# Hash-masked attention and two dense layers: transposes, value products and folds each trail the scores by one tile more

## The reference, cut to what matters

```python
q_bits = (np.einsum('bhsd,dk->bhsk', q, proj) > 0)   # k alike
mask = q_bucket[:, :, :, None] == k_bucket[:, :, None, :]
scores = np.where(mask, scale * np.matmul(q, k.transpose(0, 1, 3, 2)), -1e9)
attn = np.exp(scores - max); attn = attn / (sum + 1e-9)
x = np.matmul(attn, v)                  # to (1536, 512)
x = g1(x @ w_in1) @ w_out1              # g1: clipped square
out = (h - np.tanh(h)) @ w_out2         # h = x @ w_in2
```

## Time and profile before

| | |
|---|---|
| median of 3 runs | 764.22 us (764.16 to 764.26) |
| the profiled execution, its own time | 764.02 us |
| its span in the profile | 762.2 us |
| TensorE matmul busy (PE) | 749.6 us, 98% |
| TensorE weight load busy (PEld) | 635.6 us, 83% |
| VectorE (DVE) | 427.3 us, 56% |
| ScalarE (ACT) | 342.9 us, 45% |
| GpSimd (POOL) | 290.0 us, 38% |

### The profile page before, as it was taken

How to read it: one execution, slowest core, us unless ns; L and a number is a source line. 1 busy time by engine, 2 the same in 40 slices (tenths; PEclk the granted TensorE clock), 3 DMA queues, 4 the chain that set the end, 5 groups by cost and what they waited for, 6 DMA issues and landing times.

```text
span 762.2 us, 11644 instructions
## 1 busy us (share of the span) xinstructions
PE 749.6 (98%) x3712; PEld 635.6 (83%) x3712; DVE 427.3 (56%) x743; ACT 342.9 (45%) x679; POOL 290.0 (38%) x226
## 2 busy tenths in 40 slices
PE   5999999999999999999999999999999999999998
PEld 3889989989988888888888888888888888888886
DVE  5999999999995664343433677762221322232223
ACT  5888888888884333343333333342121312222222
POOL 6677977977989991000000465650000000000000
PEclk9999999999999999999999999999999999999999
DMA  7545445544324231000000123210000100010001
GB/s 273 149 134 144 126 130 139 134 128 133 109 77 149 70 124 56 1 0 1 1 0 1 52 86 111 83 56 1 1 0 1 55 0 0 0 55 1 1 0 56
DMA packets 21320, 50.27 MB, mean 66 GB/s; under 512 B 4814, under 2 KB 6990, under 8 KB 21290
## 3 DMA queue, kind: packets, MB, share of 16 engines
q1 hardware_dynamic: 21146, 49.47, 21.2%
q10 hardware_dynamic: 144, 0.39, 0.1%
HBM read 42.04 MB, written 3.19 MB: 59 GB/s over the span
## 4 chain that ended last, share of the span: by engine, by line
PE 85%; DVE 9%; ACT 3%; issue 2%; DMA 1%; DVEq 0%; ACTq 0%
PE ps L667 29%; PE ps L586 29%; PE ps L577 8%; PE ps L563 8%; DVE g_raw L901 5%; PE ps L549 4%; PE ps L552 4%; PE ps L505 2%; DVE g_mid L898 1%; ACT g_hi L777 1%; ACT g_mid L771 1%; DVE clamped L826 1%; DVE p_lo L843 1%; DMA qk_raw<-qk 1%; ACT probs L713 0%
## 5 line engine op out<-in xcount | busy, mean ns | idle before, releaser
L586 PE MATMUL ps<-x_hi,w 128*128 128x512 f32 (+1 forms) x768 | 251.9, 389 | 0.0
L909 DVE TENSOR_TENSOR g_lo<-g_raw,g_hi 128x512 fp32r<-128x512 f32 x96 | 70.9, 738 | 243.3 <-ACT g_hi L777 243.3
L777 ACT ACTIVATE g_hi<-g_raw 128x512 fp32r<-128x512 f32 x96 | 60.7, 632 | 289.9 <-PE ps L667 226.1
L586 PEld LDWEIGHTS ps<-x_hi,w 128*128 128x128 f32 x768 | 144.2, 188 | 29.6
L586 PE MATMUL ps<-x_lo,w 128*128 128x512 f32 (+1 forms) x384 | 149.4, 389 | 0.0
L667 PE MATMUL ps<-g_hi,w 128*128 128x512 f32 x384 | 125.8, 389 | 0.2 <-DVE g_lo L909 0.2
L667 PE MATMUL ps<-w,g_hi 128*128 128x512 f32 x384 | 118.1, 389 | 0.0
L843 DVE TENSOR_TENSOR p_lo<-ps,p_hi 128x384 fp32r<-128x384 f32 x192 | 97.9, 552 | 11.9 <-ACT p_hi L723 11.5
L367 POOL TENSOR_SCALAR w<-stage 128x1024 fp32r<-128x1024 f32 x32 | 37.3, 1166 | 164.3 <-PE ps L667 163.8
L723 ACT ACTIVATE p_hi<-ps 128x384 fp32r<-128x384 f32 x192 | 84.3, 489 | 31.2 <-PE ps L563 30.1
L826 DVE TENSOR_SCALAR_CACHE_REDUCE clamped<-ps 128x768 f32<-128x768 f32 x96 | 91.1, 950 | 1.3 <-ACT probs L713 0.6
(11 more groups left out here) (59 smaller groups left out, 854.7 us busy)
## 6 DMA issues: line engine op xcount, KB each, us to landing
stage<-weights SPq DMA_DIRECT2D x32, 512.0 KB, 3.3
q_raw<-qq SPq DMA_DIRECT2D x16, 384.0 KB, 4.0
k_raw<-kk SPq DMA_DIRECT2D x16, 384.0 KB, 4.9
qk_raw<-qk SPq DMA_DIRECT2D x15, 384.0 KB, 3.9
v_raw<-v SPq DMA_DIRECT2D x16, 192.0 KB, 4.0
inv_wide<-factors SPq DMA_DIRECT2D x16, 192.0 KB, 4.3
out<-stage SPq DMA_DIRECT2D x12, 256.0 KB, 2.1
q_a<-q_b SPq DMA_DIRECT2D x14, 192.0 KB
```

What stands on the lines that cost most here:

```text
L586: last = nc.tensor.matmul(ps[:, f % H_BANKS, :], w[:, f, wp, k * P:(k + 1) * P], xs[:, k, bass.ds(t * TOK, TOK)], start=(k == 0 and wp == ...
L777: nc.scalar.activation(g_hi[:, slot, :], g_raw[:, slot, :], ACT.Copy).then_inc(g_hi_ready, 1)
L909: nc.vector.tensor_tensor(g_lo[:, slot, :], g_raw[:, slot, :], g_hi[:, slot, :].bitcast(F32), ALU.subtract).then_inc(g_split, 1)
```

## The change

Three constants are each one larger:

```diff
-TRANSPOSE_LAG = 4
-PV_LAG = 8
-FOLD_LAG = 10
+TRANSPOSE_LAG = 5
+PV_LAG = 9
+FOLD_LAG = 11
 FACTOR_LAG = 8
 SCALE_TURNS = [8, 10]
```

## The result

The change makes the kernel slower, by more than was forecast. The median of five runs is 772.56 us (770.21 to 773.87) against 764.23 (764.16 to 765.34, five runs); the ratio is 1.0106, with a 95% interval of 1.0095 to 1.0118. The forecast was 769.7 with a range of 765.8 to 771.6, so the sign was right and the size was not. The profiled execution took 773.49 us, 9.47 more than the one of before.

The account below looks back on a forecast made before the run. Nearly full TensorE (27.98 of 27.98 us a pair) and VectorE (26.48) were taken as the bound. Terms 4.0 + 1.5 + 0 = 5.5 us on 764.02 gave 769.5, plus 0.20 for the median: 769.7 us, range 765.8 to 771.6.

Parts of the forecast that it names:

- the mechanism of the loop: Loop: scores start at the later of 2.06 us after the last scores or 1.37 after `parts_lo` two turns before.
- The fold into turn 8: Pairs 1 to 6: fold lands ahead of inversion and clamp of turn 9; 0.67 us a pair, 4.0 us.
- The fold into turn 2: Pairs 1 to 6: later fold delays inversion and the clamp of turn 3; 0.25 us a pair, 1.5 us.
- The fold into turn 11: Loop: fold moves from turn 10 with no inversion near; cost nothing, up to 0.55 us without cover.
- The prediction's own sign of being wrong: Loop: wrong if a pair stays at 28.0 us or grows in turns other than those named.
- The ramp: Pair 0 and drain: taken as nothing; at best 1.27 us returns, at worst twice a clamp's 0.95 is lost.
- The clock: Rival: pauses in the loop drop TensorE to the 1.2 GHz level, 21 us in six pairs, 785 to 790; chance 0.02.
- GpSimd: Loop: its queue comes 1.7 us later, absorbed by its 4.9 us wait, which shrinks to about 3.2; cost nothing.
- Pair 7: Last pair, without bit products: gains and losses net to about nothing, between -0.7 and +0.7 us.
- one unkind ramp: Range's upper end: the sum with 1.9 us added for a bad ramp, 771.6.
- the lesser cost: Rival: only one of the two fold places costs in full; 1.6 to 4 us, 766 to 768; chance 0.20.

Follow-up runs that it names:

- a_factor7: Changed kernel with the inversions one turn earlier, in turns 7 and 1 (FACTOR_LAG 7 instead of 8): 767.25 us, ratio 1.0024.
- b_tr5: Kernel before with the transposes alone one tile later (TRANSPOSE_LAG 5): 783.91 us, ratio 1.0250.
- a_copiesfirst: Changed kernel with SyncE's early loads reordered: bit products' rows, then second head's copies, pair 1's first head last: 770.37 us, ratio 1.0079.
- after_again: The changed kernel as it is, run again in later rounds against the kernel before: 772.37 us, ratio 1.0111.

## Why the prediction was right or wrong

**The direction and the mechanism of the loop: right.** Scores start 1.37 after `parts_lo` of two turns before, or a turn's 2.06 after the last scores. This held in the changed kernel, in the one before and in a_factor7 (pairs 1, 2 and 4), outside the turns that bit products stretch and TensorE's turns next to the jump back. In b_tr5 the waits of the value products come on top.

**The fold into turn 8: right in place and nearly in size.** Forecast 0.67 in each of six pairs; measured 0.71, so 4.3 for 4.0 us (turn 10 of six pairs, 12.61 and 16.86). The fold's own row is 0.55 us, but the next instruction stands 0.58 behind it, and the inversion took 0.50.

**The fold into turn 2: right.** Forecast and measured 0.25 a pair, 1.5 us.

**The fold into turn 11: wrong, and this is the step that failed in the loop.** The prediction said "Cost nothing", since no inversion is near and the distance to turn 2 is the same. But turn 1 grew by 0.25 on average: 13.94 us in six pairs, where it was 12.40, so 1.5 us. It took an inversion to be needed for a loss. In turn 11 the fold stands right ahead of VectorE's jump back, whose 0.19 us are added to it; the forecast did not look at the jump. Where no jump follows, behind pair 6, the move cost nothing, as forecast. A fold alone is no safe place either: in turn 8 it cost 0.25 (a_factor7). In the loop of the kernel before, TensorE's own pause of 0.2 us at its jump back came just behind the fold of turn 10 and covered it. Turns 11 and 0 got shorter by 0.46 us in all. The prediction's own sign of being wrong came true here: a pair grew in a turn that it had not named.

**The ramp: wrong, by the largest amount.** The prediction took "nothing" for it, with at worst a queue behind a later clamp. It looked at engines alone. The step that failed is that the bit products of turn 5, which do not trail, come earlier when the work ahead of them moves back. The prediction didn't ask whether their rows were there. Pair 0 and the drain are 2.85 us longer in the profiled execution: 1.92 of waiting, and the slower clock on top. The engines alone gave what was forecast: with both landings served, pair 0 is 1.62 us shorter than before and the drain 1.4 longer. By the medians of the change and a_copiesfirst the landings cost 2.0 us. Of the change's 8.3 us at the median, 6.1 are left with the landings served, nearly all in the loop.

**The clock: a rival with 0.02, which did take part.** It was priced in the loop, where pauses of 0.7 us left it at 1.00, as forecast. In pair 0 it fell behind 1.92 us without work (the change) and 2.35 us (a_factor7); it stayed at 1.00 behind 1.28 us (after_again) and 1.05 us (b_tr5). The Trainium skill ("TensorE: Matmul & The Clock Gate", Part 1) says that an idle array falls to half its clock; the trace now agrees, with a granted clock of 0.50. Three of the nine runs of the change had a mean granted clock of 0.998 or less, and they are the three longest (773.49, 773.62 and 773.87 us). No edit separates the clock's part from the wait's, so its share of the 2.0 us is not shown.

**GpSimd: right.** Its delay ended in its own wait. That shrank to 3.9 us and not to the forecast 3.2. Counted from the scores of turn 9, `scale_x` starts 2.1 us later than before, but the scores that end the wait come 1.15 us later too. **Pair 7: right**, +0.09. Its parts came as forecast: turn 5 gave back 0.72 us (3.19 to 2.47), turn 4 took 0.25, and turn 10 took 0.55, where 0.48 was forecast. Nothing in the dense layers moved: the last row's 1.37 us is what pair 0 was to give up.

**The range** ended at 771.6. It held one unkind ramp of 1.9 us and no more folds that cost. Its lower end, 765.8, is called the middle of the lesser cost, but 764.2 + 1.6 is that rival's lower end; the middle is 767.0. With the measured terms the sum is 764.2 + 4.3 + 1.5 + 1.1 + 2.0 = 773.1, within a us of the median; 1.1 is the loss in turn 1 less the gain in turns 11 and 0.

One thing stays open: turn 1 of pair 2, the first after the loop's first jump back, takes 2.5 to 2.6 us in every kernel with folds in turn 11, and 2.3 in the pairs behind it. In the change VectorE's wait ahead of that clamp is 0.48 us there, and 0.18 to 0.20 at the later jumps. Why the first one is longer is not shown.

## What to carry to other kernels

A step that trails can't be moved alone: list, for each engine's queue, which of the unmoved steps it now stands in front of, and count it as free only in a turn whose length something else already stretches. Look at the loop's jump back as a step of its own in each queue. The steps that don't trail come earlier in the ramp, so ask of each of them whether its data has landed by then. Where two engines are nearly full, an instruction of half a us may cost half of itself in each round, though its engine shows slack over the whole loop.

## What the runs showed of the hardware that I had not expected

- TensorE idle for 1.92 us in pair 0 was followed by the 1.2 GHz level: 0.66 and 0.50 granted in two stretches of 2 us. In a_factor7 it was idle for 2.35 us, and the clock 0.90, 0.50 and 0.74. After 1.28 and 1.05 us idle at the same place, the clock stayed at 1.00.
- With the DMA engines full, the same load in the same order landed anywhere from 17.41 to 19.45 us in six executions. Ahead of the 768 KB load in the queue, it landed at 13.4 to 14.0.
- The hardware loop's jump back costs about 0.2 us on TensorE (turn 11 takes 2.28 us in pair 5 and 2.06 in pair 6, which has no jump behind it; kernel before) and 0.19 on VectorE behind a fold. Each only counts where nothing else covers it.
